# Splitting the gates of the first MoE into halves, moving x's splits into the first chunk's last tiles, and taking two waits off GpSimd

## The reference

```
scores = q @ k^T / 8 ; keep those within tau of the row's maximum ; softmax ; @ v    # 32 heads, 576 x 64
x = heads laid side by side                                                          # 2304 x 512
x = ((x @ w_a) * (x @ w_b)) @ w_out        # first MoE: 512 -> 1536 -> 512
h = x @ w_in ; solu = h * softmax(h)       # second MoE: 512 -> 1024
out = (layernorm(solu) * g) @ w_out        # 1024 -> 512
```

## Time and profile before

| what | value |
|---|---|
| median of 3 runs | 977.17 us (976.65 to 977.37) |
| the profiled execution | 976.68 us |
| its span, first to last instruction | 974.6 us |
| TensorE busy | 943.8 us, 97% |
| VectorE busy | 779.4 us, 80% |
| GpSimd busy | 601.4 us, 62% |
| ScalarE busy | 508.6 us, 52% |

### The profile page before, as it was taken

The page is one execution under the profiler, slowest core; times in us unless marked ns, Lnnn a source line. Parts: engine busy times, 40 slices in busy tenths (PEclk is TensorE's granted clock), DMA queues, the critical chain, the costliest instruction groups (busy, mean ns, idle before and its releaser), DMA issues.

```text
span 974.6 us, 18670 instructions
## 1 busy us (share of the span) xinstructions
PE 943.8 (97%) x6222; PEld 869.4 (89%) x6222; DVE 779.4 (80%) x1298; ACT 508.6 (52%) x823; POOL 601.4 (62%) x570
## 2 busy tenths in 40 slices
PE   5999999999999998999999999999999999999998
PEld 5999999999998998999899999998899778888886
DVE  6778778887878577787878787877888888888884
ACT  3777777777778645333533443335434743333332
POOL 2777777777778454666576657665777754433320
PEclk9999999999999999999999999999999999999999
DMA  6666667666674564222322231123220200000001
GB/s 176 167 153 164 162 151 169 160 152 161 155 176 112 155 213 131 83 69 67 87 87 66 66 108 65 65 73 143 66 76 13 87 23 22 22 22 22 22 22 43
DMA packets 55683, 96.76 MB, mean 99 GB/s; under 512 B 15576, under 2 KB 24408, under 8 KB 55632
## 3 DMA queue, kind: packets, MB, share of 16 engines
q1 hardware_dynamic: 55632, 96.10, 35.9%
HBM read 58.41 MB, written 5.32 MB: 65 GB/s over the span
## 4 chain that ended last, share of the span: by engine, by line
PE 55%; issue 17%; POOL 13%; DVE 8%; ACT 2%; DMA 2%; SPq 1%; POOLq 0%; DVEq 0%; ACTq 0%
PE PS L1678 12%; PE PS L1640 9%; PE PS L1642 8%; POOL w_raw L739 4%; POOL w_raw L736 3%; PE PS L1837 3%; PE PS L1838 3%; PE PS L1839 3%; POOL w_raw L730 3%; PE PS L1894 3%; PE PS L1896 3%; PE PS L1895 3%; POOL w_raw L738 2%; PE PS L1705 2%; PE PS L1707 2%
## 5 line engine op out<-in xcount | busy, mean ns | idle before, releaser
L664 POOL TENSOR_TENSOR p_lo<-prob,p_hi 128x576 fp32r<-128x576 f32 x144 | 208.6, 1451 | 49.8 <-ACT p_hi L859 47.8
L1705 PE MATMUL PS<-x_parts,w_parts 128*128 128x256 f32 x672 | 191.8, 285 | 8.1 <-DVE g_parts L1332 4.2
L1640 PE MATMUL PS<-ops 128*128 128x288 f32 x642 | 182.1, 305 | 13.8 <-DVE ops L1287 6.5
L1706 PE MATMUL PS<-x_parts,w_parts 128*128 128x256 f32 x672 | 190.8, 284 | 0.0
L1707 PE MATMUL PS<-x_parts,w_parts 128*128 128x256 f32 x672 | 190.8, 284 | 0.0
L1642 PE MATMUL PS<-ops 128*128 128x288 f32 x642 | 177.5, 298 | 0.0
L1207 DVE TENSOR_REDUCE neg_max<-PS 128x1 f32<-128x576 f32 x144 | 108.5, 755 | 59.5 <-PE PS L1642 59.4
L732 POOL TENSOR_TENSOR w_parts<-w_raw,w_parts 128x768 fp32r<-128x768 f32 x48 | 90.8, 1893 | 92.4 <-ACT w_parts L986 92.4
L1640 PEld LDWEIGHTS PS<-ops 128*128 128x128 f32 x642 | 122.5, 191 | 22.7 <-issue 12.0
L1705 PEld LDWEIGHTS PS<-x_parts,w_parts 128*128 128x128 f32 x672 | 129.5, 193 | 12.2 <-DVE g_parts L1332 5.7
L1706 PEld LDWEIGHTS PS<-x_parts,w_parts 128*128 128x128 f32 x672 | 129.5, 193 | 1.8
(11 more groups left out here) (170 smaller groups left out, 2271.1 us busy)
## 6 DMA issues: line engine op xcount, KB each, us to landing
w_raw<-w_ab_dram SPq DMA_DIRECT2D x60, 512.0 KB, 3.3
qk_raw<-qkT_dram SPq DMA_DIRECT2D x32, 288.0 KB, 3.0
ops<-qk_hi SPq DMA_DIRECT2D x62, 144.0 KB
ops<-qk_hi SPq DMA_DIRECT2D x31, 288.0 KB
ops<-qk_lo SPq DMA_DIRECT2D x62, 144.0 KB
v_raw<-v_tiles_dram SPq DMA_DIRECT2D x32, 160.0 KB, 2.7
xT<-head_sb SPq DMA_DIRECT2D x32, 144.0 KB, 3.1
out_dram<-o_sb SPq DMA_DIRECT2D x18, 256.0 KB, 2.0
```

The lines of the kernel that those rows point to most:

```text
L664: pool.tensor_tensor(p_lo[:, s, :], prob[:, s, :], p_hi[:, r, :].bitcast(F32), ALU.subtract).then_inc(p_lo_done, 1)
L1640: pe.matmul(ps[:, b, 0:HALF], weights[0][:, r, own], moving[0][:, r, cols], start=(n == 0), stop=False)
L1705: pe.matmul(up_ps(bank, half), w[:, 0, :], x[:, 0, :], start=(k == 0), stop=False)
L1706: pe.matmul(up_ps(bank, half), w[:, 0, :], x[:, 1, :], start=False, stop=False)
```

## The change

Gates are split in halves of 256 columns: the first gate now stays in bank 2's second half, and its high and low parts are made in instructions of their own, with two new semaphores; part 3 of the next up waits for the first half's low part alone, part 4 for both. In chunk 0 x's second blocks and sums are split in tiles 8, 9 and 10, the weight sums after the loop, and three weight splits of tile 0 change places. GpSimd's two waits for `xs_lo_done` go. In the second MoE solu and expo_1 change places, with the two waits that follow from it, and ScalarE copies all of y's parts ahead of its second exponential. Weight sums get a semaphore of their own in place of a shared count.

```
+            expo_1 = sb(a, "expo_1", [P, F2])
             solu = sb(a, "solu", [P, F2])
-            expo_1 = sb(a, "expo_1", [P, F2])
...
-        gates_ps = PS[:, 2:4, 0:H]
+        gates_ps = (PS[:, 2, H:2 * H], PS[:, 3, 0:H])
@@ GpSimd
             with pool.Fori(1, NCH - 1) as c:
-                pool.wait_ge(xs_lo_done, 2 * c)
                 for f in range(1, NF):
                     prepare(c, f)
                 prepare(c + 1, 0)
-            pool.wait_ge(xs_lo_done, 2 * LAST_CHUNK)
@@ ScalarE, high_gates
+                act.wait_ge(up_done, UPS * (NF * c + f) + 7)
+                act.activation(half_of(g_part(0, c, f), 0), gates_ps[0], ACT.Copy).then_inc(half_hi_done, 1)
                 act.wait_ge(up_done, UPS * (NF * c + f) + UPS)
-                act.activation(in_halves(g_part(0, c, f)), gates_ps, ACT.Copy).then_inc(g_hi_done, 1)
+                act.activation(half_of(g_part(0, c, f), 1), gates_ps[1], ACT.Copy).then_inc(g_hi_done, 1)
@@ ScalarE, chunk 0
             high_wo(0)
+            high_w(2)
             high_wo(1)
-            high_w(2)
...
                 if f == NF - 1:
                     high_x_block(1, 0)
+                high_gate(f)
+                if f == NF - 4:
                     high_x_block(1, 1)
-                    high_sums(1, 0)
-                high_gate(f)
+                if f == NF - 3:
+                    high_x_block(1, 2)
+                if f == NF - 2:
+                    high_x_block(1, 3)
                 if f + 2 < NF:
                     high_w(f + 2)
                     high_wo(f + 2)
-            high_x_block(1, 2)
-            high_x_block(1, 3)
             high_blocks(1, 1)
+            high_sums(1, 0)
@@ ScalarE, second MoE
-            high_y(1, (0,))
-            act.wait_ge(y_done, LAST + 10)
+            high_y(1, (0, 1, 2))
+            act.wait_ge(y_done, LAST + 11)
             expo_step(0, 1)
-            high_y(1, (1, 2))
@@ VectorE
+            def low_half(c, f):
+                dve.wait_ge(half_hi_done, NF * (c - 1) + f + 1)
+                dve.tensor_tensor(half_of(g_part(1, c, f), 0), gates_ps[0], half_of(g_part(0, c, f), 0).bitcast(F32),
+                                  ALU.subtract).then_inc(half_lo_done, 1)
@@ products
-                done(dve.tensor_tensor(up_ps(2, 0), first, up_ps(2, 1), ALU.mult))
+                done(dve.tensor_tensor(up_ps(2, 1), first, up_ps(2, 1), ALU.mult))
                 dve.wait_ge(ab_done, n + 1)
                 done(dve.tensor_tensor(up_ps(3, 0), up_ps(3, 0), up_3[:, :], ALU.add))
+                low_half(c, f)
                 dve.wait_ge(up_done, UPS * n + 8)
                 done(dve.tensor_tensor(up_ps(3, 0), second, up_ps(3, 0), ALU.mult))
@@ VectorE, chunk 0
                 if f == NF - 1:
                     low_x_block(1, 0)
-                    low_x_sums(1, 0)
-                    low_sums(1, 0)
                 low_gate(f)
                 if f == 0:
                     low_wo(0)
+                    low_w(2)
+                    invert(last, 1)
                     low_wo(1)
-                    invert(last, 1)
-                if f + 2 < NF:
+                    low_wo(2)
+                if f > 0 and f + 2 < NF:
                     low_w(f + 2)
                     low_wo(f + 2)
-            low_x_sums(1, 1)
-            low_x_block(1, 1)
+                if f == NF - 4:
+                    low_x_sums(1, 0)
+                if f == NF - 3:
+                    low_x_sums(1, 1)
+                if f == NF - 2:
+                    low_x_block(1, 1)
+            low_sums(1, 0)
@@ VectorE, second MoE: ahead of the first solu
-                    dve.wait_ge(y_done, LAST + 11)
+                    dve.wait_ge(y_done, LAST + 10)
@@ TensorE, up
-                pe.wait_ge(g_lo_done, n)
+                if f > 0:
+                    pe.wait_ge(half_lo_done, m)
+                else:
+                    pe.wait_ge(g_lo_done, n)
                 if f == 0:
                     pe.wait_ge(xs_lo_done, 2 * c)
                 block_product(f, 5, 4, 2, 0)
                 block_product(f, 6, 1, 2, 1).then_inc(up_part, 1)
+                pe.wait_ge(g_lo_done, n)
```

More of the change, by code:

```diff
@@ L254, in build_program, with half_of @@
         UPS = 9
-        gates_ps = PS[:, 2:4, 0:H]
+        gates_ps = (PS[:, 2, H:2 * H], PS[:, 3, 0:H])
         def first_gate_of(f):
             return gate[:, f % 2 * H:(f % 2 + 1) * H]
-        def in_halves(g):
-            return g.rearrange("p (b n) -> p b n", b=2)
+        def half_of(g, half):
+            return g[:, half * H:(half + 1) * H]
         s_ps = PS[:, 0:2, :]
@@ L308, in build_program @@
         w_hi_done = sem("w_hi_done")
+        w_sum_hi_done = sem("w_sum_hi_done")
         w_sum_done = sem("w_sum_done")
@@ L326, in build_program @@
         g_done = sem("g_done")
+        half_hi_done = sem("half_hi_done")
+        half_lo_done = sem("half_lo_done")
         g_hi_done = sem("g_hi_done")
@@ L730, in prepare @@
                 pool.tensor_tensor(b12, b22, b12, ALU.subtract).then_inc(w_sum_done, 1)
-                pool.wait_ge(w_hi_done, NF + 2 * m + 1)
+                pool.wait_ge(w_hi_done, NF + m + 1)
                 pool.tensor_tensor(w_parts[:, f % 2, 1, 0:3, :], w_raw[:, f % RAW, 0:3, :],
@@ L989, in high_sums @@
                 act.wait_ge(w_sum_done, 4 * (NF * (c - 1) + f) + 4)
-                act.activation(w_parts[:, f % 2, 0, 3:7, :], w_raw[:, f % RAW, :, :], ACT.Copy).then_inc(w_hi_done, 1)
+                act.activation(w_parts[:, f % 2, 0, 3:7, :], w_raw[:, f % RAW, :, :], ACT.Copy).then_inc(w_sum_hi_done, 1)
             def copy_product(c, f):
@@ L1328, in low_gate @@
                                   ALU.subtract).then_inc(g_lo_done, 1)
+            def low_half(c, f):
+                dve.wait_ge(half_hi_done, NF * (c - 1) + f + 1)
+                dve.tensor_tensor(half_of(g_part(1, c, f), 0), gates_ps[0], half_of(g_part(0, c, f), 0).bitcast(F32),
+                                  ALU.subtract).then_inc(half_lo_done, 1)
             def low_gates(c, f):
                 dve.wait_ge(g_hi_done, NF * c + f + 1)
-                dve.tensor_tensor(in_halves(g_part(1, c, f)), gates_ps, in_halves(g_part(0, c, f)).bitcast(F32),
+                dve.tensor_tensor(half_of(g_part(1, c, f), 1), gates_ps[1], half_of(g_part(0, c, f), 1).bitcast(F32),
                                   ALU.subtract).then_inc(g_lo_done, 1)
@@ L1340, in low_sums @@
                 m = NF * (c - 1) + f
-                dve.wait_ge(w_hi_done, NF + 2 * m + 2)
+                dve.wait_ge(w_sum_hi_done, m + 1)
                 dve.tensor_tensor(w_parts[:, f % 2, 1, 3:7, :], w_raw[:, f % RAW, :, :],
@@ L1400, in low_x_sums @@
             def low_x_sums(c, part):
-                dve.wait_ge(xb_hi_done, 4 * (c - 1) + 2 + part)
+                dve.wait_ge(xb_hi_done, 4 * (c - 1) + (1 if isinstance(c, int) and c == 1 else 2) + part)
                 dve.tensor_tensor(x_parts[:, 3 + 2 * part:5 + 2 * part, 1, :, :], x_sums[:, 2 * part:2 * part + 2, :, :],
@@ L1407, in low_x_block @@
                 if part == 0:
-                    dve.wait_ge(xb_hi_done, 4 * (c - 1) + 1)
+                    dve.wait_ge(xb_hi_done, 4 * (c - 1) + (4 if isinstance(c, int) and c == 1 else 1))
                     dve.tensor_tensor(x_parts[:, 0:2, 1, :, :], xT[:, :, tokens(c, 0)].rearrange("p (b k) n -> p b k n", b=2),
@@ L1412, in low_x_block @@
                 else:
-                    dve.wait_ge(xb_hi_done, 4 * c)
+                    dve.wait_ge(xb_hi_done, 4 * c - (1 if isinstance(c, int) and c == 1 else 0))
                     dve.tensor_tensor(x_parts[:, 2, 1, :, :], xT[:, 2:4, tokens(c, 1)],
@@ L1715, in up @@
                 if f == 0:
-                    pe.wait_ge(xb_lo_done, 2 * (c - 1) + 1)
+                    pe.wait_ge(xb_lo_done, 2 * (c - 1) + (2 if isinstance(c, int) and c == 1 else 1))
                 block_product(f, 0, 0, 0, 0)
```

## The result

The changed kernel takes 981.03 us (median of 5, 980.38 to 982.14) against 977.17 (median of 5 beside it). The ratio is 1.0040, with a 95% interval of 1.0029 to 1.0051: slower by 3.9 us. Forecast were 984.0, slower.

The account below looks back on a forecast made before the run. TensorE, busy 97% of the span, bounds the kernel; its idle time and slow clock can be had. 4.4 + 3.4 − 0.8 + 0.3 = 7.3 on 976.7 gave 984.0 us, range 973.5 to 988.5.

Parts of the forecast that it names:

- Halves: At tiles 11 and 2 and in the last chunk the seven waits for gates go: up to 5.4 us gained.
- Order in tile 0: At later heads low_sums ends 4.8 us after GpSimd's last sum, so part 2 of up(1) idles 2.05 us.
- The port: VectorE and GpSimd take turns at SBUF; if not, three later heads each 1.3 us cheaper, time 980.1.
- The 0.65 us at part 4 of up(0): At later heads A22's low part waits behind GpSimd's L732, costing TensorE 0.65 us.
- GpSimd's waits: Taken out at the heads, they bring GpSimd's last sum only 0.35 us earlier; port turn-taking speaks against removal.
- Chunk 0: Tile 0's reordering gains 0.86 us, given back by tile 8; early x splits idle TensorE 2.9 us at tile 11.
- chunk 1's head: From chunk 0's tile 11 through up(1): longer idle times, one clock fall kept, +4.4 us; without any fall +2.7.
- The later heads: Three heads after chunk 1's each lose 2.7 us in place of 1.6: +1.1 each, +3.4 us.
- The last chunk's −0.8: In the last chunk two gate waits go: −0.8 us.
- the second MoE's +0.3: First transpose and ScalarE's copies of y come 0.2 to 0.3 later: +0.3 us, bounds −1 and +0.8.
- A: Rival, chance 0.20: x work and tile 0's order lie beside TensorE, the seven gate waits go: 971.3 us.
- C: Rival, chance 0.09: the clock falls at the three later heads too, 3 × 1.7 more: 989.1 us.

Follow-up runs that it names:

- e1: Changed kernel with VectorE doing tile 1's low_sums before low_half, instead of after it, in tile 0 of a chunk; 974.6 us.
- e7: Kernel before with the gates by halves alone, and low_sums of tile 1 ahead of low_half in tile 0; 974.0 us.
- e3: Changed kernel with GpSimd's two waits for the x sums put back; 988.3 us.
- e10: Kernel before with only GpSimd's two waits for the x sums taken out, gates whole; 973.6 us.
- e5: As e1, but in chunk 0's tiles 8 and 9 ScalarE copies x's sums after the weights of tile f + 2; 972.5 us.
- e8: Kernel before with only the weight splits of chunk 0's tile 2 moved ahead; 976.1 us, one run.
- e4: Kernel before with the gates by halves alone, in the changed kernel's order; 987.9 us.
- e6: As e1, with x's splits for chunk 1 back in chunk 0's tile 11 and after; 971.0 us.
- e11: As e6, with x's first pair of sums alone split early, behind the weights of tiles 10 and 11; 970.1 us.
- e9: As e6, with the second MoE's places and two waits as in the kernel before; 970.4 us.
- e2: Changed kernel with x's splits for chunk 1 back in chunk 0's tile 11 and after; 982.4 us.

## Why the prediction was right, and where its sizes were off

**Halves.** Right in mechanism: all seven waits for gates went. 0.9 to 1.0 us were gained at each tile 11 and 0.8 to 1.0 at each tile 2, as forecast (0.9 and 0.7).

**Order in tile 0.** Right, and the largest term. The time from the last sum to the end of low_sums was forecast as 4.8 us and is 4.83; TensorE's idle time at part 2 of up(1) as 2.05 and is 1.81, 1.78 and 1.71 (with the slower restart 1.97, 1.94 and 1.86). e1 and e7 show it by taking it away: 6.5 and 13.8 us, falls of the clock included. It doesn't hang on the clock: of the changed kernel's five executions two have a mean granted clock of 1.000 and took 980.4 and 980.6 us, and the kernel before's five such executions took 975.2 to 976.3.

**The port.** The 0.65 us at part 4 of up(0) is 0.36, 0.39 and 0.31 idle, 0.5 by the starts. The turn-taking was as in the earlier trace rows, L1427 waiting for L735. But as a verdict on GpSimd's waits the collisions were the small side: e3 and e10 show that the waits out gain 7.3 and 3.3 us.

**Chunk 0.** The wait at tile 11 was forecast as 2.9 and is 2.8 by the starts (2.62 idle). Of it the two copies are 1.9 (e5). The 0.9 us gained at tile 2 was to be given back by tile 8; in the table it was kept (+0.5 to −0.5). From the first down to tile 8 the changed kernel needs 29.08 us, e1 29.35 and e8 29.34, and e4, e7 and e10 with the old order 29.17 to 29.45. Only the profiled execution of the kernel before needs 30.05. GpSimd's first use of the inverse loads came 15.4 us after the first down there, 13.8 in the changed kernel and 14.5 to 14.8 in e1, e7, e8 and e10. The landing varies from run to run, so I hold this step for right, and the 1 us for chance.

**The mis-sized term, chunk 1's head.** Forecast +4.4 us, found +1.1 (from +0.5 to +1.6). 1.5 of the difference is the fall of the clock, which I kept and which didn't come here (by the starts it costs 1.5 us, from +3.1 to +1.6 in the table, and not the 1.7 that I took as half of 3.4), 1.0 the chance just told, and 0.8 the chain through tile 11 and up(0), worked out too long. The fall is worth less still in the kernel before: e8's clock stayed full there, and a wait for gates of 0.73 us came up at tile 2 of chunk 1 in its stead, so that e8 was only 0.5 us faster from there to tile 11. The later heads were forecast at +3.4 and came to +4.0, of which about 1.5 is the clock, which fell behind chunk 2's 1.81 us: without it they are +2.5, 0.9 less than forecast, since part 2 and part 4 idled somewhat less. The last chunk's −0.8 came out as −1.0 (+5.6 to +4.6), the second MoE's +0.3 as +0.1. So in the profiled execution the clock fell once, as I had said, and in another place, which is luck for the sum: with no fall at all it would have been 1.5 us less.

**Rivals.** A fails on just the point named as its decision: low_sums of tile 1 ends 4.8 us after the last sum and not within 2.7. e1 shows that with that mended and all else as changed the kernel is at 974.6, not at A's 971.3, which takes e6. C, falls at the later heads, happened at one of three in the profiled execution. The early splits of x, which A takes for covered, cost 3.5 us once the order is mended (e1 against e6).

The best found, e6 and its two variants (970.1 to 971.0), keep the halves and the waits' removal, and leave x's splits where they were, all or, in e11, all but the first pair of sums (e9 has the second MoE as before besides); they beat the kernel before by 0.64 to 0.70%.

## What to carry to other kernels

When a result is split in two so that a reader can start sooner, the cost is in the order, not in the extra instructions: a new wait in the middle of an in-order engine's sequence holds up whatever stands behind it, and there it was another product's operand with 0.3 us of slack. Look at the one iteration whose order differs from the others (here tile 0). Work moved "into idle time" goes into a serial chain if the idle engine is idle because it waits for its neighbour; place it behind what the chain hands on.

## What the runs showed of the hardware

Falls of TensorE's clock to 1.2 GHz are no function of one idle time. With TensorE idling 2.33 or 2.34 us before the same matmul of chunk 1's head, the clock fell in the profiled executions of the kernel before and of e7, and not in that of e8. At chunk 0's tile 11 it fell behind 2.63 us in e3, and not behind 2.62 in the changed kernel or 2.79 in e1. Behind 1.81 us in the changed kernel it fell; of six idle times of 3.3 us in e3 and e4 five were followed by a fall. A fall lasted 3.4 us, or 6.8 us after idle times of 3.0 (e2) and 4.8 us (e4); the five behind 3.3 us lasted 3.4, so the length doesn't follow the idle time alone either. During a fall matmuls of 256 columns start 0.21 us apart instead of 0.12, and one of 3.4 us delayed TensorE by about 1.5 us, one of 6.8 by 2.7 (e2 against e6). So a stall has a second price that comes by chance.

VectorE's subtraction with both inputs in SBUF and GpSimd's instructions took turns at their common port wherever they met in the rows shown: L735 of 1.85 us alone took 2.74 behind VectorE's L1415, and L1427 of 0.68 took 2.33 behind L735.
